# Rank matmuls of the last batch moved behind the first block's turn, and the fifth block's gather moved ahead of the third block's gates

## The reference

```python
X = np.fft.rfft(x, axis=1)                      # x: 8 x 3072 x 256
y = np.fft.irfft(X * (filt_r + 1j * filt_i)[None], n=3072, axis=1)

x = y.reshape(8 * 3072, 256)                    # then a mixture of experts, as if N = 3072
logits = x @ w_gate                             # 256 x 8
expert_idx = argmax(logits); gate_w = softmax(logits)[expert_idx]
# token by token, in order: the first 768 tokens of each expert are kept
h = relu(disp[e] @ w1[e])                       # 768 x 256 @ 256 x 1024
out[i] = gate_w[i] * (h @ w2[e])[pos[i]]        # 0 for tokens not kept
```

## Time and profile before

| | us |
|---|---|
| median of 3 runs | 492.42 |
| profiled execution, its own time | 491.62 |
| its span | 489.8 |
| PE busy | 455.6 (93%) |
| DVE busy | 233.4 (48%) |
| ACT busy | 215.3 (44%) |
| POOL busy | 186.2 (38%) |
| chain that ended last: PE, DVE | 83%, 10% |
| mean granted TensorE clock | 0.989 |

### The profile page before, as it was taken

How to read it: one execution, slowest core, us unless ns; L and a number is a source line. 1 busy time by engine, 2 the same in 40 slices (tenths; PEclk the granted TensorE clock), 3 DMA queues, 4 the chain that set the end, 5 groups by cost and what they waited for, 6 DMA issues and landing times.

```text
span 489.8 us, 12096 instructions
## 1 busy us (share of the span) xinstructions
PE 455.6 (93%) x5160; PEld 400.8 (82%) x5160; DVE 233.4 (48%) x382; ACT 215.3 (44%) x402; POOL 186.2 (38%) x159
## 2 busy tenths in 40 slices
PE   5989999997898988999979999999999999999994
PEld 5855557555665574999979999999999999999993
DVE  2085535889399965870652242353134344224300
ACT  2745555452364555622634353455335345423310
POOL 0000000000000060467476787566786457583222
PEclk9999999998999999999989999999999999999998
DMA  8994989759854365733041894411795310970001
GB/s 297 412 403 131 337 257 336 277 206 332 286 166 163 139 225 141 258 98 98 22 141 45 277 387 154 140 44 34 260 399 179 131 43 24 347 276 23 33 34 38
DMA packets 45743, 93.00 MB, mean 190 GB/s; under 512 B 5840, under 2 KB 20848, under 8 KB 45168
## 3 DMA queue, kind: packets, MB, share of 16 engines
q1 hardware_dynamic: 39408, 79.48, 46.3%
q0 software_dynamic: 6272, 12.65, 7.7%
HBM read 46.47 MB, written 45.64 MB: 188 GB/s over the span
## 4 chain that ended last, share of the span: by engine, by line
PE 83%; DVE 10%; issue 3%; DMA 2%; ACT 1%; POOLq 0%; POOL 0%; SPq 0%; DVEq 0%; ACTq 0%
PE psum L1281 29%; PE psum L1267 25%; DVE prod L791 5%; PE psum L491 4%; PE psum L508 4%; PE psum L475 4%; PE psum L548 3%; PE psum L505 3%; PE psum L646 2%; PE psum L582 2%; PE psum L538 2%; PE psum L524 1%; DVE prod L799 1%; PE psum L578 1%; DMA g_in<-y_rows,token 1%
## 5 line engine op out<-in xcount | busy, mean ns | idle before, releaser
L1095 DVE SCALAR_TENSOR_TENSOR hl<-psum,hh 128x384 fp32r<-128x384 f32 x128 | 69.5, 555 | 145.7 <-ACT hh L1046 145.7
L1281 PE MATMUL psum<-w2h,hh 128*128 128x256 f32 x384 | 110.5, 288 | 0.0
L1281 PE MATMUL psum<-w2l,hh 128*128 128x256 f32 x384 | 109.3, 285 | 0.0
L1281 PE MATMUL psum<-w2h,hl 128*128 128x256 f32 x384 | 109.3, 285 | 0.0
L1046 ACT ACTIVATE hh<-psum 128x384 fp32r<-128x384 f32 x128 | 62.1, 492 | 60.8 <-PE psum L1267 60.0
L1267 PE MATMUL psum<-xh,w1h 128*128 128x384 f32 x256 | 86.1, 336 | 1.6 <-DVE hl L1095 1.5
L1267 PE MATMUL psum<-xh,w1l 128*128 128x384 f32 x256 | 85.6, 334 | 0.0
L1267 PE MATMUL psum<-xl,w1h 128*128 128x384 f32 x256 | 85.6, 334 | 0.0
L791 DVE TENSOR_TENSOR prod<-psum,fab 128x1024 f32<-128x1024 f32 x48 | 56.5, 1217 | 49.7 <-PE psum L475 41.9
L1183 POOL DMA_INDIRECT out<-o_out,token x48 | 49.2, 1025 | 74.0 <-ACT o_out L1055 60.1
L1281 PEld LDWEIGHTS psum<-w2l,hh 128*128 128x128 f32 x384 | 74.4, 194 | 0.0
(11 more groups left out here) (111 smaller groups left out, 533.0 us busy)
## 6 DMA issues: line engine op xcount, KB each, us to landing
out<-zero SPq DMA_DIRECT2D x24, 1024.0 KB, 6.2
w_raw<-in_w SPq DMA_DIRECT2D x14, 1024.0 KB, 5.8
x_in<-in_x SPq DMA_DIRECT2D x18, 512.0 KB, 6.7
t_scratch<-t_out SPq DMA_DIRECT2D x24, 256.0 KB, 4.4
z_in<-t_scratch SPq DMA_DIRECT2D x32, 192.0 KB, 3.9
y_rows<-y SPq DMA_DIRECT2D x12, 512.0 KB, 2.8
fab<-in_fab SPq DMA_DIRECT2D x4, 1024.0 KB, 14.4
first_raw<-in_w SPq DMA_DIRECT2D x2, 1024.0 KB, 7.6
```

The lines of the kernel that those rows point to most:

```text
L1095: nc.vector.scalar_tensor_tensor(out=hl[:, b % 2, f, :], in0=ps[(2, 3, 6, 7)[f % 4]][:, 0:TOK], scalar=0.0, in1=hh[:, b % 2, f, :].bitcast ...
L1281: mm = nc.tensor.matmul(ps[4 + (b * ST + s) % 2][:, 0:D], hx[:, b % 2, f, s * P:(s + 1) * P], wt[k][:, f, :], start=(f == 0 and m == 0), s ...
```

## The change

There are two edits.

The first: the rank matmuls of the last batch go out right behind block 0's turn and ahead of the last two row products, instead of behind them. The two products go to banks 4 and 5 instead of 2 and 3, so that bank 3 is the ranks' alone. The wait for all copies of the products, which stood ahead of the ranks and so ahead of the first up matmul, is split: up group 0 waits for bank 4, up group 1 for bank 5, and a wait for banks 2 to 5 stands ahead of the first down piece.

The second: on POOL the gather of block 4 goes ahead of the gates of block 2, and loses its wait for the second up group of block 3.

```diff
--- before.py
+++ after.py
@@ -280,7 +280,7 @@
 
         psum = ctx.enter_context(nc.psum_tensor("psum", [P, 8, 2, D], F32))
         ps = [psum[:, i].rearrange("p k d -> p (k d)") for i in (0, 1, 4, 5, 2, 3, 6, 7)]
-        work = [psum[:, i].rearrange("p k d -> p (k d)") for i in range(WORK + 1)]
+        work = [psum[:, i].rearrange("p k d -> p (k d)") for i in range(6)]
         back = [psum[:, i].rearrange("p k d -> p (k d)")[:, 0:DH * 4 * HR] for i in (3, 6)]
         wide = psum[:, 4:6]
         raw_at = P
@@ -444,7 +444,7 @@
                 for n in range(NG - 1, FIRST_ZEROS):
                     zeros(sp, n)
 
-        held = [None] * (WORK + 1)
+        held = [None] * 6
         place_of = {"pe": 0, "act": 0}
 
         def next_work(engine):
@@ -648,7 +648,7 @@
 
         def place_of_row(t, i, engine):
 
-            return 2 + (i - 4) if t == HALF and i >= 4 else next_work(engine)
+            return i if t == HALF and i >= 4 else next_work(engine)
 
         def pe_last(pe, t, r):
             pe_logits(pe, t, 0)
@@ -664,11 +664,11 @@
                     for k in range(DH):
                         free_work(pe, k)
                     pe_block_turn(pe, r, 0)
+                    pe_rank(pe, t, 5)
                 pe_product(pe, t, i, place_of_row(t, i, "pe"))
-            for k in range(WORK + 1):
-                free_work(pe, k)
-            if r == 0:
-                pe_rank(pe, t, 5)
+            if r > 0:
+                for k in range(WORK):
+                    free_work(pe, k)
 
         def act_a(act, t, i, first):
             c, h = divmod(i, 2)
@@ -1225,10 +1225,9 @@
             pool_sent(pool, r, 0, range(ST - 1, ST))
             pool_gather(pool, r, 3)
             pool_sent(pool, r, 1)
+            pool_gather(pool, r, 4)
             pool_after(pool, r, 2, 6)
             pool_gates(pool, r, 2)
-            pool_after(pool, r, 3, 2)
-            pool_gather(pool, r, 4)
             pool_after(pool, r, 3, 7)
             pool_gates(pool, r, 3)
             for b in range(2, BLOCKS - 1):
@@ -1258,6 +1257,8 @@
                 for f in range(FT):
                     if n * FT + f >= 4:
                         pe.wait_ge(hl_done, n * FT + f - 3)
+                    elif n == 0 and f < 2:
+                        free_work(pe, 4 + f)
                     if b in (0, 2) and f == TURN_AFTER:
                         turn(b + 1)
                     if b == 2 and f == 3:
@@ -1293,6 +1294,9 @@
                 turn(0)
             up(0)
             up(1)
+            if r == 0:
+                for k in range(2, 6):
+                    free_work(pe, k)
             down(0, 0)
             down(0, 1)
             if r == 0:
```

## The result

The changed kernel took 486.97 us (median of 12 runs, 484.77 to 488.49), the kernel before 491.54 us (12 runs, 489.92 to 496.42) beside it. The ratio is 0.9898, with a 95% interval from 0.9874 to 0.9921: some 5 us faster, between 3.9 and 6.2. The forecast was 4.9 us, from 492.42 to 487.5. The profiled execution took 487.08 us with a span of 485.3 us (before: 491.62 and 489.8); the mean granted clock rose from 0.989 to 0.996. About half of that rise isn't the change's: from 110 to 120 us, inside the batches, the trace of before has 0.86 and the one after 1.00.

A forecast was written before the change was run, and what follows sets the result against it. TensorE bounds the kernel, held up at block 0's up half and block 4's turn: -0.8 - 4.38 + 0.3 = -4.9 us, from 492.42 to 487.5 us. Forecast's own range 486.3 to 488.7, whole range 486.0 to 490.0.

The forecast's parts named there:

- Part 1: Start of block 0's up half: ranks behind the turn bring the first up matmul 0.8 us earlier, then held by xl.
- Part 2, the wait: Block 4's turn: gather 4, issued ahead of block 2's gates, lands early, so TensorE's 2.66 us wait goes whole.
- Part 2, the clock: Behind block 4's turn: with the wait goes the slow clock (0.50) behind it, 1.72 us from turn 4 to turn 5.
- What is late next: Turn 6: POOL moves 3.0 us earlier, gather 6 lands at 285.0, wanted at 284.75; about 0.3 us wait is left.
- The sum: Whole kernel: -0.8 - 4.38 + 0.3 = -4.9 us, forecast median 487.5.
- The rule on the shared port: VectorE and GpSimd: whichever starts first holds the port pair, so the gate issue at 252.04 isn't stretched by w1l.
- rival (a): Turn 6: w1l catches the gate issue, gather 6 takes back more, wait 1.5 us: 488.7, chance 0.17; with slow clock 490.4, 0.05.
- (b): Block 0's up half: rank edit gives nothing, through another wait or VectorE late for block 1: 488.3, chance 0.07.
- (c): Turn 4: gather 4 is held on POOL's queue and lands late anyway, only the rank edit's gain left: 491.6, chance 0.03.
- (d): Turn 6: zero stores hold gather 6 longer, long wait and slow clock (1.7 us); landing at 291.5 gives 495.7; chance 0.04.

The follow-up runs named there:

- e1: The changed kernel with POOL's order of before, so only the rank edit against the kernel before; ratio to before 0.9988 (0.9953 to 1.0023).
- e6: The changed kernel with the rank matmuls behind the last two products again, new banks and split waits kept; ratio to before 0.9935.
- e3: The kernel before with 22 extra transposes on TensorE between block 3's up half and turn 4; ratio to before 0.9942 (0.9907 to 0.9977).
- e10: The changed kernel run again, unaltered, as the measure beside the late gather 6 kernel; ratio to before 0.9903 (0.9853 to 0.9952).
- e2: The kernel before with only gather 4 moved ahead of block 2's gates on POOL; ratio to before 0.9942 (0.9909 to 0.9976).
- e9: The changed kernel with three gate issues (block 6's, 3.9 us of POOL) moved ahead of gather 6; ratio to before 1.0024 (0.9996 to 1.0052).
- e11: The changed kernel with the ranks ahead of the first turn and block 0's xl ahead of w1l on VectorE; ratio to before 0.9905.
- e12: e11 with block 5's gates moved behind gather 6 and block 3's scatters on POOL, so gather 6 issues earlier; ratio to before 0.9902.
- e8: The changed kernel run again, unaltered, on a slow chip beside e6; ratio to before 0.9925 (0.9885 to 0.9964).
- e4: The changed kernel run again, unaltered, on a slow chip beside e1 and e2; ratio to before 0.9948 (0.9911 to 0.9985).

## Why the prediction was right, point by point

- **Part 1, 0.8 us.** 0.83 measured at the first up matmul, and e1 shows it alone. That it holds from there to turn 4, as the prediction has it, came out in one of four traces of the changed kernel; in the others gather 2's landing took 0.3 to 0.45 us of it. The prediction had passed over gather 2 by when it is released, which was right (30.2 us behind the first up matmul in all), and didn't ask how much room its landing had. The wait that ends last is xl, as worked out (192.22 us in the trace, the first up matmul 0.09 later). Only the account of what brings it was loose: I told the move of the ranks as the first step, and e6 shows that the same start comes without it.
- **Part 2, the wait, 2.66 us.** Turn 4 has no wait, and 24.77 - 22.22 = 2.55 us came between turn 2 and turn 4. The missing 0.1 lies in blocks 2 and 3, spread over places that I can't name.
- **Part 2, the clock, 1.72 us.** The mechanism holds (e3), the size was 0.17 too large: 1.55 by the timeline. The step that failed is reading 19.32 us in the chain of waits. Its pieces start where the piece before ends by the model, so turn 5 stands at 271.53 there and at 271.37 in the timeline, while turn 4, behind a wait, stands at 252.21 in both.
- **What is late next.** POOL moved as worked out. Seen from the first up matmul, so without part 1 and without the 0.27 us by which all was early, I had 3.0 us for gather 6; 280.90 - 276.87 = 4.03, less 0.27 and 0.83, is 2.9. The wait at turn 6 was to be 0.3 and was 0.04 in one profile and 0.17 in the other (e10).
- **The sum.** 4.88 predicted and 4.86 measured from turn 0 to turn 6. The errors (0.1 and 0.17 too much gain, 0.2 too much loss) nearly cancel, which is luck, and so is the trace: e10's has 4.47. The times say 3.9 to 6.2.
- **The rule on the shared port.** The gate issue overlapped by w1l for 0.23 us took 1.00 us, so rival (a) didn't come. The trace agrees with what the Trainium skill (SBUF — State Buffer, on the shared port pair) says of the one that starts first, as far as one overlap of that kind can tell.
- **The rivals.** (b) is excluded at the first up matmul by e1, (c) at turn 4 by e2. (d) didn't happen, but e9 shows its price, and that it was at most 3.9 us of POOL away. I gave it too small a price: behind a wait of 4.2 us the clock cost 2.4 us and not 1.7.

## What to carry to other kernels

Price a wait of TensorE at its length plus what the clock loses behind it (here 1.55 us behind 2.66, but nothing behind the pause of 1.01 us in block 3's up half), and read both between starts of one timeline, not from the chain. When a wait goes, follow the queue of the engine that feeds the next stages through the whole shift, with every stretched issue and loaded landing: it told turn 6 to 0.3 us here. A feed that arrives just in time makes the traces differ by its landing: e11 and e12 are 0.5 us apart at turn 2 with the same program up to there, so a gain of that size wants more than one trace. And when matmuls wait for a buffer, first ask whether they need it; their place in the order may not matter.

## What the runs showed of the hardware

The slow clock cost more behind the longer of two waits: 1.55 us behind 2.66 us without work, 2.4 us behind 4.2. The two lie at different places, so the length isn't shown to be the reason. It came on at different times: in e9 the stretch from 287.8 to 289, still inside the wait, has 0.68, while before the change the clock was 1.00 until 253 and fell 1.4 us after work had begun again at 252.21 (its stretch from 253 to 254 has 0.83; if the clock fell once from 1.00 to 0.50, that was at 253.7).

```profile
253.00:254.00 1.00, 1.00 (x9) 1.00 (x9) 0.69 (x2) 1.00 (x3) 0.69 (x2) 0.83 0.02 1
```

Chips differ more than the change is worth. On two of the chips the medians of all kernels were 503 to 512 us, on the others 486 to 493. On the two slow ones the traces show ScalarE and TensorE standing at three places, the same in all kernels (between turns 2 and 3, 5 and 6, 14 and 15). How long they stand differs: turn 2 to turn 3 takes 12.6 to 16.1 us there (9.8 on the others), so the ratios of e1 to e8 carry this scatter too. One of them in ScalarE's timeline of e4:

```profile
276.97 0.48 ACT L1055 ACTIVATE o_out<-psum,o_gate 128x256 f32<-128x256 f32 x1 [2.62 <-PE psum L1282]
287.88 0.84 ACT L1055 ACTIVATE o_out<-psum,o_gate 128x256 f32<-128x256 f32 x2 [10.43 <-remote]
```

"remote" means that the profile knows no releaser. The instruction waits for down matmuls that by TensorE's own records were some 8 us before. What holds the signal back I can't say; the instruction queues moved as many packets as on the other chips (43, and 20 or 21). It stays open.
